# Moving GpSimd's weight splits and one weight cast to other blocks of a windowed attention

## The reference

```python
scores = scale * np.matmul(q, k.transpose(0, 1, 3, 2)) + bias      # bias = -slope(head) * distance
scores = np.where(is_global | is_local, scores, -1e9)
a = np.exp(scores - np.max(scores, axis=-1, keepdims=True))
a = a / (np.sum(a, axis=-1, keepdims=True) + 1e-09)
x = np.matmul(a, v)                                                # (1536 tokens, 512)
h = x @ w_in                                                       # w_in 512 x 2048
g = (a0 + a1*h + a2*h**2 + a3*h**3) / (1 + |b0|*|h| + |b1|*h**2 + 1e-6)
x = g @ w_out                                                      # 2048 -> 512
```

## Time and profile before

| | |
|---|---|
| time, median of 3 runs | 483.35 us (483.05 to 484.37) |
| the profiled execution | 483.05 us, its span 481.0 us |
| TensorE busy | 469.4 us, 98% |
| VectorE busy | 378.1 us, 79% |
| ScalarE busy | 271.7 us, 56% |
| GpSimd busy | 55.5 us, 12% |

### The profile page before, as it was taken

How to read it: one execution, slowest core, us unless ns; L and a number is a source line. 1 busy time by engine, 2 the same in 40 slices (tenths; PEclk the granted TensorE clock), 3 DMA queues, 4 the chain that set the end, 5 groups by cost and what they waited for, 6 DMA issues and landing times.

```text
span 481.0 us, 7546 instructions
## 1 busy us (share of the span) xinstructions
PE 469.4 (98%) x2734; PEld 383.1 (80%) x2734; DVE 378.1 (79%) x705; ACT 271.7 (56%) x481; POOL 55.5 (12%) x123
## 2 busy tenths in 40 slices
PE   7899899999999999999999999999999999999997
PEld 5676678888888878888888888888888888888885
DVE  6998989999999989777889999999685555555550
ACT  6999998656656465455555545443554333333341
POOL 4768870000000000000000000000000000000000
PEclk9999999999999999999999999999999999999999
DMA  8998864000000000000033446331012222222201
GB/s 293 326 360 293 337 236 178 1 0 1 0 1 1 0 1 0 1 1 0 1 96 102 131 128 170 113 94 44 1 44 67 66 65 65 66 69 76 72 23 44
DMA packets 25665, 42.91 MB, mean 89 GB/s; under 512 B 2080, under 2 KB 16800, under 8 KB 24480
## 3 DMA queue, kind: packets, MB, share of 16 engines
q1 hardware_dynamic: 23760, 36.64, 22.0%
q0 software_dynamic: 1296, 5.24, 3.7%
q10 hardware_dynamic: 576, 0.60, 0.4%
HBM read 33.04 MB, written 3.15 MB: 75 GB/s over the span
## 4 chain that ended last, share of the span: by engine, by line
PE 85%; ACT 5%; DVE 4%; POOL 4%; issue 1%; DMA 0%; DVEq 0%; ACTq 0%; POOLq 0%
PE ps L1197 9%; PE ps L1198 9%; PE ps L1199 9%; PE ps L1128 8%; PE ps L1129 8%; PE ps L1130 8%; PE ps L1260 5%; PE ps L1262 5%; PE ps L1261 5%; PE ps L1217 5%; PE ps L1215 5%; PE ps L1216 5%; ACT probs L480 3%; POOL probs L442 2%; PE ps L1243 2%; PE ps L1094 1%
## 5 line engine op out<-in xcount | busy, mean ns | idle before, releaser
L1197 PE MATMUL ps<-gate_hi,bank_b_hi 128*128 128x512 f32 x192 | 74.9, 390 | 0.5 <-DVE tok_lo L941 0.5
L1128 PE MATMUL ps<-tok_hi,bank_a_hi 128*128 128x512 f32 x192 | 75.1, 391 | 0.0
L1129 PE MATMUL ps<-tok_lo,bank_a_hi 128*128 128x512 f32 x192 | 74.8, 389 | 0.0
L1130 PE MATMUL ps<-tok_hi,bank_a_lo 128*128 128x512 f32 x192 | 74.7, 389 | 0.0
L1198 PE MATMUL ps<-gate_lo,bank_b_hi 128*128 128x512 f32 x192 | 74.7, 389 | 0.0
L1199 PE MATMUL ps<-gate_hi,bank_b_lo 128*128 128x512 f32 x192 | 74.7, 389 | 0.0
L542 ACT ACTIVATE quad<-ps 128x1024 f32<-128x1024 f32 x23 | 23.6, 1028 | 57.8 <-DVE rest L879 57.8
L480 ACT ACTIVATE probs<-negs,small 128x256 f32<-128x256 f32 (+1 forms) x96 | 46.0, 483 | 1.6 <-DVE small L725 1.3
L442 POOL TENSOR_SCALAR probs<-probs,small 128x256 f32<-128x256 f32 (+1 forms) x96 | 42.4, 460 | 18.2 <-DVE small L736 18.1
L861 DVE SCALAR_TENSOR_TENSOR quad<-quad,small,absh 128x1024 f32<-128x1024 f32 x23 | 29.5, 1282 | 18.0 <-ACT absh L545 17.8
L1197 PEld LDWEIGHTS ps<-gate_hi,bank_b_hi 128*128 128x128 f32 x192 | 36.0, 188 | 8.7 <-issue 1.2
(11 more groups left out here) (103 smaller groups left out, 948.2 us busy)
## 6 DMA issues: line engine op xcount, KB each, us to landing
v_sb<-in_v_win SPq DMA_DIRECT2D x8, 704.0 KB, 6.1
bank_a_raw<-in_w_in SPq DMA_DIRECT2D x4, 1024.0 KB, 7.9
bank_b_raw<-in_w_out SPq DMA_DIRECT2D x4, 1024.0 KB, 7.2
stage_hi<-tok_hi SPq DMA_DIRECT2D x12, 256.0 KB, 2.7
stage_lo<-tok_lo SPq DMA_DIRECT2D x12, 256.0 KB, 2.8
out_dram<-out_sb SPq DMA_DIRECT2D x12, 256.0 KB, 2.0
q_sb<-in_q_t SPq DMA_DIRECT2D x14, 192.0 KB, 5.0
k_sb<-in_k_win SPq DMA_DIRECT2D x7, 384.0 KB, 6.8
```

The costliest lines, as they stand in the source:

```text
L1128: pe.matmul(banks(bank, 1), bank_a_hi[:, f, ws], x_hi, start=(k == 0), stop=False)
L1129: pe.matmul(banks(bank, 1), bank_a_hi[:, f, ws], x_lo, start=False, stop=False)
L1130: mm = pe.matmul(banks(bank, 1), bank_a_lo[:, f, ws], x_hi, start=False, stop=(k == KT - 1))
L1197: pe.matmul(banks(4 + k, 1), bank_b_hi[:, f, ws], g_hi, start=first, stop=False)
```

## The change

The cast goes from block 7 to block 8. The splits go from the list (20, 22, 32, 34) to every sixth block from 15: 15, 21, 27 and 33. The loads, the number of GpSimd's tiles and all instructions stay as they are, and the other branch of the program (other window sizes) is untouched.

```diff
--- before.py
+++ after.py
@@ -245,8 +245,8 @@
     LAG = 4
     GROUPS = FT // 2
     N_GROUPS = CHUNKS * GROUPS
-    POOL_IN, SPLITS_AT = 4, (20, 22, 32, 34)
-    LOADS_AT, CAST_AT = (1, 3, 4, 5), 7
+    POOL_IN, SPLIT_FROM, SPLIT_EVERY = 4, 15, 6
+    LOADS_AT, CAST_AT = (1, 3, 4, 5), 8
     LATE_IN = FT - 4
     IDLE_IN, END_IN = POOL_IN + 5, LATE_IN - 1
 
@@ -442,8 +442,9 @@
                     pool.tensor_scalar(pv, pv, prec[n // 2 % (PB // 2)][:, j:j + 1], 1.0, ALU.mult, ALU.mult).then_inc(probs_ready, 1)
                 if n == CAST_AT:
                     cast_w_in()
-                if n in SPLITS_AT:
-                    split_in_low(SPLITS_AT.index(n))
+                f, part = divmod(n - SPLIT_FROM, SPLIT_EVERY)
+                if part == 0 and 0 <= f < POOL_IN:
+                    split_in_low(f)
         with pool.Else():
             cast_w_in()
             for f in range(POOL_IN):
```

## The result

| | runs | time, median | range | granted clock |
|---|---|---|---|---|
| before | 14 | 483.20 us | 482.98 to 485.27 | not on record for these |
| changed | 14 | 486.62 us | 484.33 to 490.15 | 0.992 to 0.996 |
| changed, the profiled execution | 1 | 483.23 us | | 1.000 |

The ratio of changed to before is 1.0065, with a 95% interval of 1.0046 to 1.0085: slower, where I forecast no measurable change at 483.85 us. The profiled execution behaves quite differently from the timed ones: it is 3.4 us shorter than their median, and it is the only one of the fifteen with a mean granted clock of 1.000.

What follows compares the result with a forecast made beforehand. ScalarE and VectorE together were taken to bound the attention stage. Gain -2.0, w_in wait +2.5 and later pairs +0.1 gave +0.6 at most; +0.5 on 483.05 made 483.55, plus 0.3 for the median 483.85; range 482.3 to 485.0 us.

Steps and rivals of the forecast that it cites:

- the mid-pair stalls: Attention stage: splits in the middle of a pair delay VectorE and ScalarE; moving them between pairs gains 2.0 us.
- rival A: Block 15: w_in is there in time or the wait is hidden, so only the gain stays, -1.7 us, 481.65; chance 0.13.
- the first period: Attention stage, 16.71 to 32.23 us: 15.52 us for twelve blocks; the two later ones lose 1.27 and 0.73 against it.
- The next pairs' 0.1 us at blocks 21 and 33: Splits after blocks 21 and 33 start the next pair late, mostly covered; 0.1 us put for both together.
- do no more work: Second and third attention stretches: ScalarE and VectorE work no more than in the first, yet show idle time.
- A split at 15 waits for w_in, and the wait takes the place of the gain: After block 15 GpSimd waits for raw w_in, holding up pair 16: +2.5 us against the -2.0 gain.
- All of the cast still lies ahead of w_in's end, so w_in lands at about 31.3 ... not later than 32.25: Cast issued 1.75 us later, 0.32 MB displaced at 0.42 MB/us: w_in lands 0.8 us later; bounds 29.9 to 32.25.
- No row here shows a fall: Granted clock 1.00 in every stretch of the kernel before, longest TensorE idle 1.09 us; said against rival C.
- rival C: TensorE idle about 2.0 us before pair 16 lowers its clock to 1.2 GHz: +2.4 to +4.8 us, about 487; chance 0.03.

Runs made afterwards that it cites:

- e1: The kernel before with only its four splits moved, to after blocks 21, 23, 33 and 35; cast still after block 7: 482.05 us, ratio 0.9978.
- e10: The changed kernel with the cast back after block 7 and splits after 21, 27, 33 and 39: 481.24 us, ratio 0.9950.
- e12: The changed kernel with the first raw w_in load issued earlier and the cast back after block 7: 481.03 us, ratio 0.9949.
- e8: The changed kernel itself run once more, to trace an execution like the timed ones: 487.03 us, ratio 1.0076.
- e14: The changed kernel with the cast after block 9 instead of 8: 486.51 us, ratio 1.0059.
- e11: The changed kernel with w_in loaded early, cast after block 7, and GpSimd held after block 15 by ten unused multiplications: 487.01 us, ratio 1.0063.
- e9: The changed kernel with only the cast put back after block 7: 483.13 us, ratio 0.9989.
- e13: The changed kernel with the cast after block 6 instead of 8: 482.93 us, ratio 1.0004.
- e6: The changed kernel with w_in loaded early and GpSimd held after block 15 by four unused multiplications: 482.70 us, ratio 0.9992.

## Why the prediction was wrong

**What bounds the stage, and what the mid-pair stalls cost.** Right. e1, e10 and e12 had no wait at block 15 and no low clock but one: their ratios of 0.9978, 0.9950 and 0.9949 are -1.1, -2.4 and -2.5 us where I wrote -2.0 (and -1.7 for rival A, in which the data is there in time). I took the first period, 15.52 us, as the measure of both later ones. In e10, without stalls, they take 15.54 and 15.00 us, so each had lost 1.25 us, 2.5 together. The next pairs' 0.1 us at blocks 21 and 33 was too small to be seen. That VectorE and ScalarE "do no more work" in the later stretches is not quite what the earlier trace rows say: in the second they are busy 0.21 and 0.54 us longer.

**A split at 15 waits for w_in, and the wait takes the place of the gain.** Right in kind and, in the profiled execution, in size: start at 31.25 (forecast 31.3), pair 16 at 32.51 (32.6), one wait of 2.19 us (about 2.5), total +0.2 us against the profiled execution before (+0.5).

**"All of the cast still lies ahead of w_in's end, so w_in lands at about 31.3 ... not later than 32.25".** This step failed, first in time. I moved the cast's bytes and kept the rate at 0.42 MB/us. In the kernel before, the cast's packets had the transfer engines nearly alone until 22 us. When the cast starts later, the loads of q and k are ahead of it, and once its packets move, both queues are under way side by side for several microseconds. In e8 fewer bytes get through as well (272 GB/s against 403), in e14 hardly (388); why is not shown. The cast's transfer takes 5.0 to 5.4 us after block 6 or 7 (5.9 and 6.4 with the early load) and 8.5 to 10.6 after block 8 or 9. w_in's, issued at its old place, takes 8.6 to 9.4 us with the first and 9.8 to 11.7 with the second. In e8 the landing was at 34.2 us, or 32.9 with the later start taken off, beyond my bound, and VectorE's wait was 4.05 us. In e14 it was at 32.1, just inside the bound, and the time was still 485.82: a late landing alone is not the whole miss.

**"No row here shows a fall": the clock, rival C at 0.03.** This step failed too: the sum has no term for the clock. I had it as a rival, with the right mechanism and a price too high (+2.4 to +4.8; the stretch with the low clock was 1.40 us longer in e8 and 1.63 in e14), but gave it almost nothing because no row of before showed a fall. The forecast itself put TensorE in a gap twice as long as any in that trace, so its rows could not speak for a clock of 1.00. A chance of 0.03 was far too small. The Trainium skill's page "TensorE: Matmul & The Clock Gate", section "Why this matters for your kernels", warns that idle gaps between bursts of matmuls lower the clock. The traces of e14, e8 and e11 agree, with the clock at 0.50 after gaps of 3.08, 3.36 and 4.02 us.

**The two failures are one chain.** The late landing makes TensorE's gap longer (3.36 us in e8, 2.06 in the profiled execution, 1.52 in e9), and a gap of three to four microseconds brings the clock down (e14, e8, e11). All seventeen timed executions of the changed kernel had a low clock, e9's, with the cast back and the earlier landing, four of twelve.

What stays open: why the profiled execution of the changed kernel escaped (w_in's transfer took 10.0 us there, 11.7 in e8), why fewer bytes get through in e8, and why half of e13's executions had a low clock; no run separates these. Of the executions without a trace only time and clock are known, so that their landings were late is inferred from e8, e14 and the medians. The longest, 490.15 us, is not accounted for. That the profiled execution, at 483.23, lies close to the forecast is not a success of the forecast: its landing was as I had put it, and it is the exception.

## What to carry to other kernels

A transfer's rate is not a constant that moves with it: before a load is moved, look at which other queue's packets are under way at its new place, and let the landing's upper bound include a lower rate. Compare the time and the clock of the profiled execution with the timed ones before its trace is read as theirs. When a forecast makes TensorE wait longer than it ever does in the trace at hand, that trace says nothing about the clock there, and the wait's price must include the fall. And put helper work between pairs, after its data has landed: the same four splits after 21, 27, 33 and 39 save 0.5% (ratio 0.9950, 0.9930 to 0.9970) where starting at 15 with a later cast loses 0.65%.

## What the runs showed of the hardware

A clock fall does not need a long gap every time. In e6's profiled execution it followed a gap of 1.15 us and slowly fed transposes (busy 1.56 of the 2 us from 32 to 34), while the kernel before has a gap of 1.09 us near 13 us and its granted clock is 1.00 from 12 to 16 us. Three more of e6's twelve executions had a low clock, but where it fell in them is not known. Once down, TensorE's clock was at 0.50 for nearly seven microseconds in e8 (worked out from the rows of 34 to 42 us), though TensorE was busy again from 36.16 us on.
